# A fused attention, gated-MLP and routed-expert kernel: the first projection tile's h split moved beside the last gate/value chunks, and the last two tiles' steps reordered

## The reference, cut to what matters

```
h    = silu(x @ w_gate) * (x @ w_val)       # 1536 x 1536, the gate/value stage
x1   = h @ w_out                            # 1536 x 512,  the projection
skip = x1 @ w_skip > 0                      # routing, per token
e    = argmax(x1 @ w_gate2); gate = softmax(x1 @ w_gate2)[e]
out  = x1, and where skip: x1 + gate * (relu(x1 @ w1[e]) @ w2[e])    # 8 experts
```

## Time and profile before

| | |
|---|---|
| time, median of three runs | 586.46 us (585.88 to 586.92) |
| the profiled execution | 585.22 us, of which the span of the trace is 583.3 us |
| mean granted TensorE clock | 0.972 of full speed |
| TensorE busy | 94% of the span |
| gate/value stage | to 285.7 us |
| projection | from 290.0 to about 412.8 us |
| experts | from 424.3 us to the end |

### The profile page before, as it was taken

How to read it: one execution, slowest core, us unless ns; L and a number is a source line. 1 busy time by engine, 2 the same in 40 slices (tenths; PEclk the granted TensorE clock), 3 DMA queues, 4 the chain that set the end, 5 groups by cost and what they waited for, 6 DMA issues and landing times.

```text
span 583.3 us, 10567 instructions
## 1 busy us (share of the span) xinstructions
PE 546.4 (94%) x3752; PEld 461.8 (79%) x3752; DVE 240.3 (41%) x671; ACT 180.7 (31%) x419; POOL 95.3 (16%) x136
## 2 busy tenths in 40 slices
PE   7899999999999999999799999999189998999994
PEld 5677777888888888888588888888089997999993
DVE  5777761333332333232313435441635144155311
ACT  4677862111111011111212424331313133144110
POOL 2234457200111111000000010101101111102111
PEclk9999999999999999999889999999579999999998
DMA  7888522111011111000150113651554677845111
GB/s 213 231 281 232 157 97 76 56 54 53 12 43 54 54 54 54 0 0 1 62 244 36 55 54 132 264 198 55 181 199 180 243 299 296 319 177 189 64 37 36
DMA packets 29509, 73.55 MB, mean 126 GB/s; under 512 B 2816, under 2 KB 15104, under 8 KB 25376
## 3 DMA queue, kind: packets, MB, share of 16 engines
q1 hardware_dynamic: 26592, 63.61, 31.7%
q0 software_dynamic: 2880, 9.47, 4.8%
HBM read 61.77 MB, written 11.29 MB: 125 GB/s over the span
## 4 chain that ended last, share of the span: by engine, by line
PE 88%; DVE 4%; DMA 4%; issue 2%; ACT 1%; POOL 0%; DVEq 0%; POOLq 0%; ACTq 0%
PE bank L1382 12%; PE bank L1223 11%; PE bank L1225 11%; PE bank L1227 11%; PE bank L1297 6%; PE bank L1301 6%; PE bank L1299 6%; PE bank L1209 4%; PE bank L1394 3%; PE bank L1396 3%; PE bank L1395 3%; PE bank L1186 3%; PE bank L1165 2%; DMA w_raw<-w 2%; PE bank L1317 1%
## 5 line engine op out<-in xcount | busy, mean ns | idle before, releaser
L1223 PE MATMUL bank<-x_hi,w_hi 128*128 128x512 f32 x288 | 112.2, 390 | 0.4 <-issue 0.4
L1227 PE MATMUL bank<-x_hi,w_lo 128*128 128x512 f32 x288 | 112.1, 389 | 0.0
L1225 PE MATMUL bank<-x_lo,w_hi 128*128 128x512 f32 x288 | 112.0, 389 | 0.0
L1382 PEld LDWEIGHTS bank<-xgT,w_sb 128*128 128x128 f32 x704 | 82.8, 197 | 1.9 <-issue 1.2
L1382 PE MATMUL bank<-xgT,w_sb 128*128 128x128 f32 x704 | 83.0, 280 | 0.8 <-ACT xgT L757 0.8
L953 DVE TENSOR_TENSOR sig<-sig,bank 128x512 f32<-128x512 f32 x36 | 24.8, 688 | 130.3 <-ACT sig L677 130.3
L677 ACT ACTIVATE sig<-bank 128x512 f32<-128x512 f32 x36 | 21.5, 598 | 162.7 <-PE bank L1227 162.7
L1223 PEld LDWEIGHTS bank<-x_hi,w_hi 128*128 128x128 f32 x288 | 54.1, 188 | 11.9 <-issue 0.8
L1297 PE MATMUL bank<-wo_hi,hh_hi 128*128 128x512 f32 x144 | 59.3, 412 | 4.3 <-DVE hh_lo L974 4.3
L1227 PEld LDWEIGHTS bank<-x_hi,w_lo 128*128 128x128 f32 x288 | 54.1, 188 | 11.3
L1225 PEld LDWEIGHTS bank<-x_lo,w_hi 128*128 128x128 f32 x288 | 54.1, 188 | 11.1
(11 more groups left out here) (140 smaller groups left out, 711.9 us busy)
## 6 DMA issues: line engine op xcount, KB each, us to landing
w_sb<-w SPq DMA_DIRECT2D x16, 1024.0 KB, 6.5
w_raw<-w SPq DMA_DIRECT2D x16, 1024.0 KB, 8.3
w_raw<-w_gv SPq DMA_DIRECT2D x12, 512.0 KB, 3.4
va_sb<-v_long SPq DMA_DIRECT2D x10, 512.0 KB, 3.6
xg<-expert_rows POOLq DMA_DIRECT2D x13, 257.0 KB, 2.9
vb_sb<-v_tail SPq DMA_DIRECT2D x10, 320.0 KB, 4.8
q_sb<-qT SPq DMA_DIRECT2D x12, 256.0 KB, 5.1
k_sb<-kT SPq DMA_DIRECT2D x12, 256.0 KB, 6.2
```

What stands on the lines that cost most here:

```text
L1223: nc.tensor.matmul(ps[:, :], w_hi[:, u, a, k, :], x_hi[:, k, tok], start=(k == 0), stop=False)
L1225: nc.tensor.matmul(ps[:, :], w_hi[:, u, a, k, :], x_lo[:, k, tok], start=False, stop=False)
L1227: last = nc.tensor.matmul(ps[:, :], w_lo[:, u, a, k, :], x_hi[:, k, tok], start=False, stop=(k == KD - 1))
L1382: last = nc.tensor.matmul(ps, w1_sb[u][:, k, fc], xgT[:, k * P:k * P + P], start=(k == 0), stop=(k == KD - 1))
```

## The change

Three things. First, the two halves of tile 0 are split to homes of their own, `first_hi` and `first_lo` in area 3 over `w_raw` and `wo_raw`, between chunks 0 and 1 of slice 11. So `wo_raw`, `w_hi`, `w_lo` and `sig` change places in area 3, ScalarE waits there for `w_lo_made` and the `h_ready` of chunk 0, VectorE for `wo_made`. The split of tile 1 follows on ScalarE as soon as the last gate/value matmul is done, and the split of tile 2 comes ahead of copy_rows(0). Second, SyncE issues `w2` of expert 0 first and `w1` of expert 0 only after the first projection tile is in PSUM. Third, tiles 10 and 11 leave TensorE's loop; logits(10) stand in the middle of the second half of tile 11, ranks(10) ahead of columns(11), and exp_logits(10) ahead of copy_rows(11).

```diff
         w_raw = place("w_raw", (P, 2, 2, KD, P), 3, 0)
-        w_hi = place("w_hi", (P, 2, 2, KD, P), 3, 8, F32R)
-        w_lo = place("w_lo", (P, 2, 2, KD, P), 3, 16, F32R)
-        sig = place("sig", (P, 2, CH), 3, 24)
-        wo_raw = place("wo_raw", (P, 2, DM), 3, 28)
+        wo_raw = place("wo_raw", (P, 2, DM), 3, 8)
+        w_hi = place("w_hi", (P, 2, 2, KD, P), 3, 12, F32R)
+        w_lo = place("w_lo", (P, 2, 2, KD, P), 3, 20, F32R)
+        sig = place("sig", (P, 2, CH), 3, 28)
+        first_hi, first_lo = place("first_hi", (P, FT1, P), 3, 0, F32R), place("first_lo", (P, FT1, P), 3, 6, F32R)
...
             sp.wait_ge(wo_made, FT1)
+            load_w2(0)
+
+            sp.wait_ge(rows_in_psum, 1)
             load_w1(0)
-            load_w2(0)
...
-            slice_of_h(FT1 - 1, 1)
+            slice_of_h(FT1 - 1, 1, range(1))
...
+            a.wait_ge(w_lo_made, 2 * FT1)
+            a.wait_ge(h_ready, SLICES - NCH + 1 + FREE_GV)
+            split_h(0, 0, first_hi)
+            slice_of_h(FT1 - 1, 1, range(1, NCH))
...
             a.wait_ge(gv_ready, SLICES)
+            split_h(1, 1)
             a.wait_ge(h_ready, SLICES + FREE_GV)
-            split_h(0, 0)
-            split_h(1, 1)
+            split_h(2, 0)
             copy_rows(0, 0, 16)
-            split_h(2, 0)
             copy_columns(0)
...
             for t in range(NT // 2, NT + 1):
+                if t == NT:
+                    exp_logits(t - 2, t % 2)
                 copy_rows(t - 1, (t - 1) % 2, ((t - 1) // 2) * 16 + 16)
                 if t + 1 < NT:
                     split_h(t + 1, (t + 1) % 2)
-                exp_logits(t - 2, t % 2)
+                if t < NT:
+                    exp_logits(t - 2, t % 2)
...
+            d.wait_ge(wo_made, FT1)
+            split_h(0, 0, first_hi, first_lo)
+            slice_of_h(FT1 - 1, 1, range(1, NCH))
...
-            split_h(0, 0)
             split_h(1, 1)
             split_h(2, 0)
...
-            rows_of_x1(0, 0, 0)
-            rows_of_x1(0, 0, 1)
+            for q in range(2):
+                rows_of_x1(0, 0, q, hi=first_hi, lo=first_lo)
             tile_of_x1(1, 1, first=True)
-            with pe.Fori(1, NT // 2) as j:
+            with pe.Fori(1, NT // 2 - 1) as j:
                 tile_of_x1(j * 2, 0)
                 tile_of_x1(j * 2 + 1, 1)
+            tile_of_x1(NT - 2, 0)
+            rows_of_x1(NT - 1, 1, 0)
+            columns_of_x1(NT - 2, 0)
+            ranks(NT - 3, 1)
+            rows_of_x1(NT - 1, 1, 1, range(FT1 // 2, FT1 - 3))
+            logits_of_x1(NT - 2)
+            rows_of_x1(NT - 1, 1, 1, range(FT1 - 3, FT1))
+            ranks(NT - 2, 0)
             columns_of_x1(NT - 1, 1)
-            ranks(NT - 2, 0)
             logits_of_x1(NT - 1)
             ranks(NT - 1, 1)
```

More of the change, by code:

```diff
@@ L672, in _, with slice_of_h @@
                 hold(a, "act")
-            def slice_of_h(f, u):
-                for c in range(NCH):
+            def slice_of_h(f, u, chunks=range(NCH)):
+                for c in chunks:
                     a.wait_ge(gv_ready, f * 3 + c + 1)
@@ L967, in _, with split_h @@
                     slice_of_h(f, u)
-            slice_of_h(FT1 - 1, 1)
-            def split_h(t, u):
+            slice_of_h(FT1 - 1, 1, range(1))
+            def split_h(t, u, hi=None, lo=None):
                 for q in range(2):
@@ L1288, in _, with rows_of_x1 @@
             pe.wait_ge(wr_in, 16)
-            def rows_of_x1(t, u, q):
+            def rows_of_x1(t, u, q, fs=None, hi=None, lo=None):
+                fs = range(q * FT1 // 2, (q + 1) * FT1 // 2) if fs is None else fs
                 pe.wait_ge(h_split, t * 2 + q + 1)
-                if q == 0:
+                if fs[0] == 0:
                     pe.wait_ge(x1_ready, t - 1 + FREE_OUT)
-                for f in range(q * FT1 // 2, (q + 1) * FT1 // 2):
-                    nc.tensor.matmul(out_ps[u][:, :], hh_hi[:, u, f, :], wo_hi[:, f, :], start=(f == 0), stop=False,
+                for f in fs:
+                    h_hi = hh_hi[:, u, f, :] if hi is None else hi[:, f, :]
+                    h_lo = hh_lo[:, u, f, :] if lo is None else lo[:, f, :]
+                    nc.tensor.matmul(out_ps[u][:, :], h_hi, wo_hi[:, f, :], start=(f == 0), stop=False,
                                      skip_group_check=True)
-                    nc.tensor.matmul(out_ps[u][:, :], hh_hi[:, u, f, :], wo_lo[:, f, :], start=False, stop=False,
+                    nc.tensor.matmul(out_ps[u][:, :], h_hi, wo_lo[:, f, :], start=False, stop=False,
                                      skip_group_check=True)
-                    last = nc.tensor.matmul(out_ps[u][:, :], hh_lo[:, u, f, :], wo_hi[:, f, :], start=False,
+                    last = nc.tensor.matmul(out_ps[u][:, :], h_lo, wo_hi[:, f, :], start=False,
                                             stop=(f == FT1 - 1), skip_group_check=True)
-                if q:
+                if fs[-1] == FT1 - 1:
                     last.then_inc(rows_in_psum, 1)
```

9 lines of the change are left out of this document (5 added, 4 removed).

## The result

The changed kernel took **577.41 us** (median of 5 runs, 577.24 to 578.9), the kernel before 585.88 us (5 runs, 585.46 to 586.92): a ratio of 0.9859, 95% interval 0.9843 to 0.9875, so 1.4% faster. The forecast was 579.8 us with 577.7 to 582.3 as its range. The five runs of before include the three of the forecast, whose median was 586.46.

A forecast was written before the change was run, and what follows sets the result against it. TensorE, busy 94% of the span, was taken to bound the kernel, gaining only from less waiting or a higher clock. -4.45 - 2.45 + 0.2 = -6.7 us from the 586.46 median gave 579.8 us, range 577.7 to 582.3.

The forecast's parts named there:

- Part 1: Between gate/value stage and projection: splitting tile 0 beforehand saves 4.45 us of waiting and 2.45 of slow clock, together 6.90 us.
- The rival in which the hole only moves: Tile 1's halves come late, TensorE empties after tile 0 and loses the clock as before: 586.7 us, chance 0.05.
- the one in which the clock's cost stays: Only the wait ahead of the projection goes, TensorE still pays for 1.2 GHz: 582.2 us, chance 0.06.
- the term for the clock: Start of the projection: twelve matmuls at half clock take 5.17 us, at full clock 2.72, so 2.45 us saved.
- The microsecond either way: Projection start: the clock's return varies between runs, so the sum would carry about a microsecond either way.
- The cost of the tail: Last projection tiles: with logits(10) moved, copy_rows(11) and all behind it come 0.2 us later.
- the loads decide: Ahead of the experts, TensorE's nine register loads end 1.2 us after the gathered tile lands and set the start.
- The experts start 6.7 us earlier: Expert stage: it starts 6.7 us earlier, at half clock as before.
- The median moves with the profiled execution: Whole kernel: profiled 585.22 us lay 1.24 below the median, so 6.7 was taken from 586.46, giving 579.8.
- The "slower" rival: TensorE's unrolled last two tiles wait for instructions in tile 10, 8.3 us plus 2.45 of low clock: 590.6 us, chance 0.04.
- The tail pays: Ahead of the experts, shorter register loads give -2.0 us in place of +0.2: 577.6 to 577.8 us, chance 0.07.

The follow-up runs named there:

- e3: Kernel before plus 18 useless matmuls on TensorE in the hole ahead of the projection, so the clock stays up: 583.23 us against 586.01, ratio 0.9929.
- e2: Kernel before with only the reordered projection tail of TensorE and ScalarE, first tile as before: 585.50 us, ratio 0.9982.
- g1: Kernel before plus 102 matmuls in a branch never taken, moving only TensorE's later code: 584.88 us against 586.04, ratio 0.9985.
- e1: Changed kernel with the old tail on TensorE and ScalarE (first tile's split, homes and SyncE's order only): 579.13 us against 586.01, ratio 0.9876.
- h2: Changed kernel with the old tail, 102 never-run matmuls, and useless transposes keeping TensorE at work ahead of the experts: 576.65 us, ratio 0.9837.
- h3: Changed kernel with the old tail and 102 matmuls in a branch never taken: 577.73 us against 587.04, ratio 0.9853.
- e4: The changed kernel run again, no line different: 579.55 us, ratio 0.9865.
- g2: Changed kernel plus 26 matmuls in a branch never taken, moving only TensorE's later code: 578.42 us, ratio 0.9856.
- g4: Changed kernel plus 90 matmuls in a branch never taken: 578.12 us, ratio 0.9852.
- i1: Changed kernel plus 82 useless transposes ahead of the experts and 46 matmuls in a branch never taken: 575.17 us against 585.15, ratio 0.9811.
- g3: Changed kernel plus 64 matmuls in a branch never taken: 578.99 us, ratio 0.9864.

## Why the prediction was right, and where it was not

**Part 1 was right in each step.** The first projection matmul came one step behind the last gate/value one (285.54, forecast 285.57). The clock stayed at its full level, worth 2.3 to 2.5 us by e3 (forecast 2.45). The added split left 1.72 us on ScalarE and 1.16 on VectorE (forecast 1.7 and 1.1). Tile 1 was in time. SyncE's wait ended at 293.89 with tile 0 in PSUM, and nobody waited for what stood behind it. In all -6.96 us against -6.90. The rival in which the hole only moves, and the one in which the clock's cost stays, are both excluded by these rows; the term for the clock was the trace's own. The three profiles that have the hole (before, e2 and g1) each show 6.8 us at half clock and take 15.5 to 15.7 us from the last gate/value matmul to copy_rows(0). The Trainium skill ("TensorE: Matmul & The Clock Gate", Part 1) puts the change to full clock within half a microsecond either way from run to run. The microsecond either way that I had made of it does not show in these profiles.

**The cost of the tail was right in size, in part by luck.** Up to copy_rows(11) it was +0.28 against +0.2. But before, at 106.5 us, is the shortest of all profiles in this stretch: the five others with the old order (e1, e3, g1, h2, h3) have 106.6 to 107.0, and the new order has 106.8 in seven of eight. What the new order shows is a steady time, TensorE and no longer GpSimd deciding it, and e2 (107.2, GpSimd deciding after all) is the exception. The whole reordering is worth nothing by h3 against the changed kernel. The step "the loads decide" held, by 0.1 to 0.2 us in place of the 1.2 that I had counted, because the gather took 5.16 us where it had taken 3.85; nine loads took 0.2 us less in all, which is the -0.20 of the first table. In e4 and h3 the gather landed last, and there the stretch is 17.7 and 17.4 us; in the other nine profiles without fillers in this place it is 16.6 to 17.1. What makes this gather late in some was not settled.

**"The experts start 6.7 us earlier", and nothing about them changes: this step failed.** The sum had no term for the experts, and they became 0.9 us shorter. I had weighed TensorE's new straight code for one thing only, a stall of TensorE itself in tile 10, and found it unlikely; there was none. What I did not ask is where the code behind it goes. It moves by some 205 instructions, a packet of it leaves the middle of a gather's flight, the gather takes 4.7 us and not 5.7, SyncE's loads go out 0.9 us earlier, w2 is whole 1.1 us earlier, and TensorE's stall for it shrinks from 1.86 us to 0.78: -0.9 us. G1 and g2 show it by moving the code alone, both ways. The Trainium skill ("Runtime: NRT & Kernel Launch", Instruction fetch mechanics) says that code comes in blocks of 16 KB by the sequencer's own DMA queue and that crossing from one to the next is mostly hidden. The size agrees (16.4 KB a packet here), and no wait of TensorE in these traces was traced to missing code. But a transfer beside the packet paid 1.0 us for it.

**"The median moves with the profiled execution" failed too.** I put the result 1.24 us above what the profile's sum gave, because the median of before lay there. The profiled execution of before was one without the fall of the clock in the attention stage. In a set of 17 later runs of before the five at a mean clock of 0.972 have a median of 585.0 us and the nine at 0.969 or 0.97 one of 586.4, so a median of three depends on which kind is among them. Of the five runs of after three had the profiled one's mean clock, 0.979 (the others 0.977 and 0.976), and their median is the profiled time itself. Against the spans alone the sum misses by 7.8 - 6.7 = 1.1 us, of which the experts are 0.9 and the tail 0.1. Of the 2.4 us between 579.8 and 577.41 the other 1.3 are this step. When the same kernel was run again (e4) it gave 579.55. Which kind a set of runs falls into is not the kernel's doing, as far as these runs show; the range should have held it on both sides.

The "slower" rival priced a stall that never came. "The tail pays" had 577.6 to 577.8, next to what was measured, but by luck: its mechanism, shorter register loads worth 2.0 us, gave 0.2.

## What to carry to other kernels

A hole that one engine's split or copy leaves in TensorE's work costs twice, its length and the slow stretch behind it; both can be read from the trace of before and add up to within 0.1 us, and filling the hole with useless matmuls shows the second cost by itself. When an edit adds or removes code on an engine, ask where all code behind it goes: a microsecond in an untouched stage is within reach of one instruction packet, and a variant with dead code of the same length separates that from the edit's own effect. When a load goes out in halves, compare first half with first half: the chain of waits names whichever ended last on its way. And when an engine waits for two things, look up the end of each: the bracket names only one of them. Before a profiled execution is set against a median, see which kind of execution it was, and keep the distance between the two as part of the range and not as a shift.

## What the runs showed of the hardware that was not expected

- A packet of instructions for one engine slows other transfers. One of 16.4 KB in the middle of a 257 KB gather's flight goes with 5.5 to 5.7 us in place of 4.7 (four profiles, before, e1, e3 and g2, against six, after, e2, e4, g1, g4 and i1), though q8 holds only 3.1% of the 16 engines in those 2 us. It is not the only thing that does: in g3 the gather took 6.1 us without one. Code that is never run shifts such packets as well as code that is.
- 4.29 us of idle TensorE after dense work brought 6.8 us at 1.2 GHz; a hole of 12 us, with only scattered matmuls in the 5 us ahead of it, brought 20.5. Fillers of 128x512 matmuls kept the clock at 1.00 throughout; 128x128 transposes kept it at 1.00 from 409 on, with 3.4 us at half clock ahead of that.
- The granted clock also falls once in the attention stage, in some executions and not in others, with TensorE at work: the windows of 15 to 30 us have 1.00 in before, after, g1, g4 and h3 and 0.89 in the other nine profiles, with 13.07 us of busy TensorE in each.
